# Two buffers for moments and normalised x, q and k split a step sooner, operands made one by one, and weight sums on VectorE in an attention and mixer kernel

## The chip, the cores and the metric

The kernel runs on one core of a Trainium2 chip. What is measured is the device time of one execution, in microseconds. The profile and the trace are of one further execution that the hardware profiler recorded.

## What is computed

Three parts follow each other, in fp32: attention with normalised q and k over 4 batches and 12 heads (448 rows, 64 columns a head), then a block of two matrices with a ReLU between them behind a layer norm, then the same kind of block behind a low-rank mixing along the rows.

```python
q_n, k_n = rmsnorm(q, g_q), rmsnorm(k, g_k)
attn = softmax(q_n @ k_n.T / sqrt(64))                 # 48 heads of 448 x 448
x = (attn @ v)                                         # as 4 x 448 x 768
xn = (x - mean) / sqrt(var + 1e-06) * g_ln
x = x + relu(xn @ w_ch1) @ w_ch2                       # 768 -> 3072 -> 768
u = x + (x.transpose(0, 2, 1) @ U @ V).transpose(0, 2, 1)   # rank 32
out = u + relu(u @ w_ch1b) @ w_ch2b
```

## The kernel before, in words

**Attention.** Two heads are a pair; there are 24 pairs, six for a batch, and each pair is worked in four steps n = 4t + i of 112 rows, so there are 96 steps and 6 that drain. TensorE's order in a step is fixed: the scores of step n (L643), for both heads the product with v of step n - 2 (L663) and the transposes of the exponentials of step n - 1 (L651); after them, where i = 2, the transposes of the next pair's normalised K (L631, `turn_k`), and in some steps those of a finished x or of a normalised x (L674, `turn_x`). All transposes go to two scratch banks in PSUM, sc_ps, taken in turn; the engine that reads a bank frees it. ScalarE copies the first head's transposes, makes the exponentials, and splits q and k (`q_high`, `k_high`: the part that fits the faster matmul format; the rest is q_lo and k_lo, and a product takes three matmuls, hi x hi, hi x lo, lo x hi). VectorE takes the maximum (L951), multiplies it into a bias (L957), makes k_lo (L943) where i = 3, copies the second head's transposes (L962), and does the sums for the norms. GpSimd squares q and k (L517, `squares`, where i = 3), takes the power -1/2 (L523, `root`, i = 0), scales K and makes q_lo (`norm_k` and `q_low`, i = 2). x of a pair stays in one of seven buffers until the statistics of its batch's six pairs are combined (`aggregate`, L990, on VectorE, where i = 3 of the pair after the batch's last), a root is taken (`root_var`) and GpSimd or, at the end, VectorE has normalised it (`normalise`). `XN_AT` says in which step a normalised x is transposed; ScalarE scales it into st_n (`keep_norm`) and SyncE stores it in HBM as xnrm.

**The four stages.** Stages 0 and 1 are the first block for two batches each, stages 2 and 3 the second. A stage has 156 products in a list `prods` (the steps end as the list begins): six times two groups of seven (kind "G", L696) and twelve of kind "M" (L706). The seven products P1 to P7 multiply sums of quarters of the weights by sums of quarters of the input (the scheme of Strassen and Winograd), and VectorE combines them. A product's weights are split by ScalarE (`weight_high`, four products ahead) and VectorE (`weight_low`, three ahead). Four of a group's seven need a sum of weights, made by GpSimd at places given by `sums_at`, five, five, four and zero products before, from the group's first: L579. For the first group of all, these places fall between the attention's last steps: the list `seq` has ("pre", -5) after step 58 and ("pre", -4) after step 59.

**Making operands.** Before a stage its input is loaded as three sets of four quarter tiles (c = 0 to 2: into `make0` in stage 0, into make_a, make_b and ht after), and from each set GpSimd makes four differences in place, ScalarE seven high parts (in_hi) and VectorE seven low parts (in_lo, L1012). `make_at` lays these out: ten consecutive places a set, of which the first is the load of all four tiles, which share one semaphore. For stage 0 the places begin at steps 66, 77 and 88 less the two of the load; for the others at the last M's first product, and 3 and 5 after it. In stages 1 and 2 the low-rank mixing runs beside the products, in twelve items, six for each pair of batches, 22 products apart from the tenth product on (`MIX_FROM`): load, transposes, products, and a store that the loads of stage 2 and 3 wait for.

What sets the order is each engine's own queue: every engine walks the list `seq` and issues what its own block puts at a place, and semaphores do the rest. The waits that the change touches are these:

```python
def aggregate(b):                                  # VectorE
    wait(dve, norm_done, PB * b)                   # moments has one buffer
def keep_norm(t):                                  # ScalarE
    wait(act, xn_out, 16 * t)                      # st_n has one buffer
def load_made(s, c):                               # SyncE, stages 2 and 3
    sp.wait_ge(mx_out, 32 * ITEMS * (s - 1))       # all of the mixing
```

## Time and profile before

| | us |
|---|---|
| median of 3 runs | 1830.38 (1827.22 to 1836.04) |
| the profiled execution, time | 1818.59 |
| its span in the trace | 1816.8 |
| PE busy in the span | 1772.3 (98%) |
| DVE busy | 1121.1 (62%) |
| ACT busy | 683.0 (38%) |
| POOL busy | 495.3 (27%) |

PE is TensorE, DVE VectorE, ACT ScalarE, POOL GpSimd and SP SyncE, whose queue issues the DMAs. Times in the trace count from the span's start. A busy TensorE need not be one at its peak: it runs at 2.4 or at 1.2 GHz, and the granted clock, 1.00 or 0.50 or between them in a stretch that has both, stands beside the windows. "[3.35 <-DVE e_t L962]" behind an instruction means that its engine sat idle so long before it and what ended that. L with a number is a line of the kernel.

### The profile page before, as it was taken

Reading aid. Unit: us, or ns where it says so; the run is one execution under the profiler, and the core shown is the slowest. Engines: PE = TensorE matmul, PEld = TensorE weight load, DVE = VectorE, ACT = ScalarE, POOL = GpSimd, SP = SyncE. Lnnn points to the kernel's source line nnn. Section 1 sums busy time; section 2 is a strip of 40 time slices with the busy share of each in tenths; the row PEclk is TensorE's granted clock in tenths of the full one; section 3 lists DMA queues with packets and bytes.
Section 4 is the critical chain, followed back from the end, with each engine's and each line's share of the span. In section 5 each row is a group of like instructions: output and inputs, shape, how many; then the busy total and the mean of one; then the engine's idle time right before and its main releaser. Section 6 shows DMA issues by size and latency. Waiting matters only on the chain.

```text
span 1816.8 us, 27033 instructions
## 1 busy us (share of the span) xinstructions
PE 1772.3 (98%) x9972; PEld 1598.1 (88%) x9972; DVE 1121.1 (62%) x2088; ACT 683.0 (38%) x1588; POOL 495.3 (27%) x419
## 2 busy tenths in 40 slices
PE   9999999999999999999999998999999989999999
PEld 8888777878999999899998897998888979999998
DVE  5787655586555565865655568566545694555554
ACT  4666544465233322433222334333223242333221
POOL 5556664364111111411110115111111151011110
PEclk9999965588999999999999999999999999999999
DMA  3222221221221211432222214322222252212112
GB/s 110 65 79 78 72 87 57 72 77 66 66 88 63 70 53 53 164 135 89 73 73 73 73 62 160 138 73 74 71 73 73 78 182 91 70 53 70 46 59 79
DMA packets 54738, 149.28 MB, mean 82 GB/s; under 512 B 5984, under 2 KB 36832, under 8 KB 54608
## 3 DMA queue, kind: packets, MB, share of 16 engines
q1 hardware_dynamic: 54608, 147.55, 24.7%
q8 instruction: 81, 1.33, 0.3%
q14 instruction: 49, 0.40, 0.1%
HBM read 122.75 MB, written 24.77 MB: 81 GB/s over the span
## 4 chain that ended last, share of the span: by engine, by line
PE 87%; DVE 8%; POOL 2%; DMA 1%; issue 1%; ACT 1%; SPq 0%; DVEq 0%; ACTq 0%; POOLq 0%
PE mm_ps L706 35%; PE mm_ps L696 31%; PE mm_ps L663 9%; PE mm_ps L643 4%; PE sc_ps L651 4%; DVE in_lo L1012 3%; PE sc_ps L674 1%; POOL x_nat L586 1%; DVE acc L1052 1%; DVE w_lo L1003 1%; PE sc_ps L718 1%; POOL qk_sq L517 1%; PE mm_ps L743 1%; DMA xres<-xa 1%; DVE h_lo L1019 1%
## 5 line engine op out<-in xcount | busy, mean ns | idle before, releaser
L706 PE MATMUL mm_ps<-h_hi,w_hi 128*128 128x448 f32 x1152 | 424.0, 368 | 10.3 <-DVE w_lo L1003 9.7
L706 PE MATMUL mm_ps<-h_hi,w_lo 128*128 128x448 f32 x1152 | 421.6, 366 | 0.0
L706 PE MATMUL mm_ps<-h_lo,w_hi 128*128 128x448 f32 x1152 | 421.6, 366 | 0.0
L1052 DVE TENSOR_TENSOR acc<-mm_ps,acc 128x448 f32<-128x448 f32 x288 | 166.3, 619 | 364.1 <-PE mm_ps L706 364.1
L696 PE MATMUL mm_ps<-in_hi,w_hi 128*128 128x448 f32 x1008 | 372.1, 369 | 2.3 <-DVE w_lo L1003 1.2
L696 PE MATMUL mm_ps<-in_hi,w_lo 128*128 128x448 f32 x1008 | 368.5, 366 | 0.0
L696 PE MATMUL mm_ps<-in_lo,w_hi 128*128 128x448 f32 x1008 | 368.4, 365 | 0.0
L825 ACT ACTIVATE w_hi<-w_raw 128x256 fp32r<-128x256 f32 (+1 forms) x480 | 205.7, 452 | 212.8 <-PE mm_ps L706 187.7
L706 PEld LDWEIGHTS mm_ps<-h_hi,w_hi 128*128 128x128 f32 x1152 | 216.5, 188 | 29.8 <-DVE w_lo L1003 11.6
L706 PEld LDWEIGHTS mm_ps<-h_hi,w_lo 128*128 128x128 f32 x1152 | 216.7, 188 | 17.8
L706 PEld LDWEIGHTS mm_ps<-h_lo,w_hi 128*128 128x128 f32 x1152 | 216.8, 188 | 17.3
L1003 DVE TENSOR_TENSOR w_lo<-w_raw,w_hi 128x256 fp32r<-128x256 f32 (+1 forms) x480 | 231.0, 493 | 0.2
L663 PEld LDWEIGHTS mm_ps<-v,e_t 112*112 112x112 f32 x1536 | 192.3, 202 | 34.7 <-issue 27.1
L663 PE MATMUL mm_ps<-v,e_t 112*112 112x64 f32 x1536 | 209.4, 287 | 0.0
L696 PEld LDWEIGHTS mm_ps<-in_hi,w_hi 128*128 128x128 f32 x1008 | 189.6, 188 | 18.9 <-DVE w_lo L1003 3.7
L696 PEld LDWEIGHTS mm_ps<-in_hi,w_lo 128*128 128x128 f32 x1008 | 189.5, 188 | 15.4
L862 ACT ACTIVATE h_hi<-ht 128x448 fp32r<-128x448 f32 x144 | 83.4, 579 | 317.1 <-DVE ht L1037 175.2
L696 PEld LDWEIGHTS mm_ps<-in_lo,w_hi 128*128 128x128 f32 x1008 | 189.6, 188 | 14.4
L579 POOL TENSOR_TENSOR w_s<-w_raw 128x384 f32<-128x384 f32 x48 | 57.5, 1198 | 501.9 <-DMA w_raw<-in_w 431.9
L579 POOL TENSOR_TENSOR w_s<-w_raw,w_s 128x384 f32<-128x384 f32 x48 | 49.4, 1029 | 506.7 <-DVE w_lo L1003 506.7
L791 ACT ACTIVATE e_nat<-mm_ps,nbias,rs 112x448 f32<-112x448 f32 x192 | 136.9, 722 | 6.6 <-DVE nbias L957 6.6
L951 DVE TENSOR_REDUCE nmax<-mm_ps 112x2 f32<-112x896 f32 x96 | 104.7, 1091 | 52.2 <-PE mm_ps L643 51.4
(104 smaller groups left out, 2040.1 us busy)
## 6 DMA issues: line engine op xcount, KB each, us to landing
w_raw<-in_w SPq DMA_DIRECT2D x96, 768.0 KB, 4.4
qk<-in_qkv SPq DMA_DIRECT2D x24, 448.0 KB, 3.8
acc<-xres SPq DMA_DIRECT2D x6, 1344.0 KB, 9.7
qt_raw<-in_q_t SPq DMA_DIRECT2D x24, 224.0 KB, 2.5
v<-in_qkv SPq DMA_DIRECT2D x24, 224.0 KB, 2.6
xnrm<-st_n SPq DMA_DIRECT2D x24, 224.0 KB, 1.9
xres<-acc SPq DMA_DIRECT2D x24, 224.0 KB, 2.2
xa<-xres SPq DMA_DIRECT2D x24, 224.0 KB, 2.7
```

The lines of the kernel that those rows point to most:

```text
L579: nc.gpsimd.tensor_tensor(out, in0, in1, op).then_inc(sum_done, 1)
L643: last = nc.tensor.matmul(mm_ps[:TP, 2 * (n % 2) + h, :S], a[rows, t % 2, i * TP:(i + 1) * TP], b[rows, t % 2], start=a is q_hi and b is k ...
L651: last = nc.tensor.transpose(to[:TP, c * TP:(c + 1) * TP], e_nat[:, n % 3, h, c * TP:(c + 1) * TP], ident[:TP, :TP])
L663: last = nc.tensor.matmul(mm_ps[:TP, 4 + t % 2, cols], e_t[h][:, c * TP:(c + 1) * TP], v[:, t % 2, h, c], start=c == 0, stop=c == NI - 1)
L696: last = nc.tensor.matmul(bank(q), w[a][:, c * P:(c + 1) * P], x[:, k, c], start=k not in ONTO and c == 0 and p == 0, stop=c == HC - 1 and ...
L706: last = nc.tensor.matmul(bank(q, b), w[a][:, c * P:(c + 1) * P], x[:, half, 2 * c + b], start=half == 0 and c == 0 and p == 0, stop=half ...
L791: nc.scalar.activation(e_nat[:, n % 3, h], mm_ps[:TP, 2 * (n % 2) + h, :S], ACT.Exp, bias=nbias[:, n % 2, h:h + 1], scale=rs[:, t % 2, 0, ...
L825: nc.scalar.activation(w_hi[:, q % RING, :width(q)], weights(q), ACT.Copy).then_inc(whi_done, 1)
L862: nc.scalar.activation(h_hi[:, g % 2, h], src, ACT.Relu).then_inc(hhi_done, 1)
L951: nc.vector.reduce_max(nmax[:, n % 2], mm_ps[:TP, 2 * (n % 2):2 * (n % 2) + 2, :S], axis=AX, negate=True).then_inc(max_done, 1)
L1003: nc.vector.tensor_tensor(w_lo[:, q % RING, :w], weights(q), w_hi[:, q % RING, :w].bitcast(F32), ALU.subtract).then_inc(wlo_done, 1)
L1052: nc.vector.tensor_tensor(acc[:, b, d], bank(q, b), acc[:, b, d], ALU.add).then_inc(ev_done, 1)
```

## The change

Several things are changed together. moments, var4 and rstd4 have two buffers by the batch's parity, and the waits are for the batch before the last. st_n has two buffers with a semaphore each. `XN_AT` has the transposes of normalised x only in steps with i = 0 or 1. `q_high` is issued at i = 1 instead of 2, and `k_high` at the end of i = 2 instead of the start of i = 3; `root_var` and `normalise` follow the buffers. `make_at` is replaced by four lists, one each for loads, sums, highs and lows: each tile has its own load and semaphore, each sum its own place, and for stage 0 no high part is made at i = 3. For stages 1 to 3 the order in which operands are made is P1, P7, P5, P3, P2, P6, P4, and the places spread from 10 products before the last M to 11 after. The loads of stages 2 and 3 wait for the mixing item that wrote their tile alone. `MIX_FROM` is 4 instead of 10, and the wait for all low parts before a mixing item is gone. The sums of weights are issued by VectorE at the same places, `weight_sum` ahead of `weight_low`. The shortened diff:

```diff
-    make_at = {}
-    for c, first in enumerate((66, 77, 88)):
-        for off in range(-2, 8):
-            make_at.setdefault(("step", first + off + off // 3), []).append((0, c, off))
+    MADE = ((P1, P3, P2, P5, P7, P6, P4), (P1, P7, P5, P3, P2, P6, P4))
+    load_made_at, sum_made_at, high_made_at, low_made_at = {}, {}, {}, {}
+    slots = [n for n in range(65, N) if n % NI != NI - 1][:7 * HC]
+    for c in range(HC):
+        at = slots[7 * c:7 * c + 7]
+        for k, n in zip(MADE[0], at):
+            high_made_at.setdefault(("step", n), []).append((0, c, k))
+            low_made_at.setdefault(("step", n + (n % NI == 2)), []).append((0, c, k))
+        for k, n in ((P5, at[1]), (P7, at[1]), (P6, at[2]), (P4, at[3])):
+            sum_made_at.setdefault(("step", n), []).append((0, c, k))
+        for tile in range(4):
+            n = 63 if c == 0 else slots[7 * c - 7 + (3, 4, 6, 5)[tile]] + 1
+            load_made_at.setdefault(("step", n), []).append((0, c, tile))
     for s in range(1, STAGES):
         first = number["M", s - 1, NJ - 1, 0]
-        for c in range(HC):
-            for off in range(-2, 8):
-                make_at.setdefault(("prod", first + (0, 3, 5)[c] + off), []).append((s, c, off))
-    MIX_FROM, MIX_STEP, ITEMS = 10, 22, 2 * HC
+        for c, ats in enumerate(((-5, -3, -1, 1, 2, 4, 6), (-4, -2, 0, 2, 3, 6, 10), (5, 7, 8, 8, 9, 10, 11))):
+            for k, n in zip(MADE[1], ats):
+                high_made_at.setdefault(("prod", first + n - 1), []).append((s, c, k))
+                low_made_at.setdefault(("prod", first + n), []).append((s, c, k))
+            for k, n in ((P5, ats[0]), (P7, ats[0]), (P6, ats[3]), (P4, ats[4])):
+                sum_made_at.setdefault(("prod", first + n), []).append((s, c, k))
+            for tile in range(4):
+                load_made_at.setdefault(("prod", first + (-10, -8, 2)[c]), []).append((s, c, tile))
+    MIX_FROM, MIX_STEP, ITEMS = 4, 22, 2 * HC
...
-            XN_AT[4 * (PB * (b + 1) + 2) + ((0, 4, 8, 12, 16, 20), (0, 2, 4, 6, 8, 10), (0, 4, 8, 12, 14, 16))[b][c]] = t
+            XN_AT[4 * (PB * (b + 1) + 2) + ((0, 4, 8, 12, 16, 20), (0, 1, 4, 5, 8, 9), (0, 4, 8, 12, 13, 16))[b][c]] = t
...
-                def load_made(s, c):
+                def load_made(s, c, n):
+                    b, cc = 2 * (s % 2) + n % 2, c + n // 2 * HC
                     if s == 0:
-                        sp.wait_ge(xn_out, 16 * (PB + HC + c + 1))
+                        u = PB * b + cc
+                        sp.wait_ge(xn_out[u % 2], 16 * (u // 2 + 1))
                         if c:
-                            sp.wait_ge(inlo_done[c - 1], made(0, P4))
+                            sp.wait_ge(inlo_done[c - 1], made(0, (P5, P7, P4, P6)[n]))
+                            sp.wait_ge(tin_done[c - 1], 4)
                     else:
+                        sp.wait_ge(inlo_done[c], made(s - 1, P4))
...
-                            sp.wait_ge(mx_out, 32 * ITEMS * (s - 1))
-                            sp.wait_ge(inlo_done[c], made(s - 1, P4))
+                            sp.wait_ge(mx_out, 32 * (ITEMS * (s - 2) + HC * (n % 2) + cc // 2 + 1))
                         if c == 2:
                             sp.wait_ge(hlo_done, 4 * NG * s)
+                    sp.dma_start(make_tiles(s, c)[:, n], (xnrm if s < 2 else xres)[b, cc]).then_inc(make_in[c][n], 16)
...
-                                all_made(sp, prods[n][1] + 1)
...
                 def root_var(b):
                     pool.wait_ge(var_done, b + 1)
-                    nc.gpsimd.tensor_tensor(rstd4[:], var4[:], m_half[:TP, :NI], ALU.pow).then_inc(rstd_done, 1)
+                    wait(pool, norm_done, PB * (b - 1))
+                    nc.gpsimd.tensor_tensor(rstd4[:, b % 2], var4[:, b % 2], m_half[:TP, :NI], ALU.pow).then_inc(rstd_done, 1)
...
+                def make_sum(s, c, k):
                     b11, b12, b21, b22 = (make_tiles(s, c)[:, x] for x in range(4))
+                    for n in {P5: (0, 1), P7: (3,), P6: (), P4: (2,)}[k]:
+                        pool.wait_ge(make_in[c][n], 16 * (s + 1))
+                    wait(pool, tin_done[c], 4 * s + SUMS.index(k))
+                    if k in (P5, P6, P4):
+                        pool.wait_ge(inlo_done[c], made(s, {P5: P1, P6: P3, P4: P2}[k]))
+                    out, in0, in1 = {P5: (b11, b12, b11), P7: (b12, b22, b12), P6: (b22, b22, b11),
+                                     P4: (b21, b21, b22)}[k]
+                    nc.gpsimd.tensor_tensor(out, in0, in1, ALU.subtract).then_inc(tin_done[c], 1)
...
-                            for u in (xn_pair(n + 1), xn_pair(n + 3)):
+                            for u in (xn_pair(n + 1), xn_pair(n + 2)):
...
-                    wait(act, xn_out, 16 * t)
-                    nc.scalar.activation(st_n[:], scratch("n", t)[:, :S], ACT.Copy,
+                    wait(act, xn_out[t % 2], 16 * (t // 2))
+                    nc.scalar.activation(st_n[t % 2][:], scratch("n", t)[:, :S], ACT.Copy,
...
-                        if i == 3 and t + 1 < NP_:
-                            k_high(t + 1)
...
+                        if i == 1 and t + 1 < NP_:
+                            q_high(t + 1)
                         if i == 2 and t + 1 < NP_:
-                            q_high(t + 1)
+                            k_high(t + 1)
...
-                    wait(dve, norm_done, PB * b)
+                    wait(dve, norm_done, PB * (b - 1))
...
+                def weight_sum(r, k):
+                    weights_in(dve, r)
...
+                    nc.vector.tensor_tensor(out, in0, in1, op).then_inc(sum_done, 1)
...
+                    for r, k in sums_at.get(n, ()):
+                        weight_sum(r, k)
                     for q in low_at.get(n, ()):
                         weight_low(q)
```

## Rows read from the trace of the kernel before

**Rows 1.** The page's 40 slices of the span: granted TensorE clock in tenths.
```profile
PEclk9999965588999999999999999999999999999999
```

**Rows 2.** Windows of attention: from:to, length, busy (xinstructions) by engine, granted clock, DMA.
```profile
14.00:200.00 186.00, 184.05 (x1681) 155.62 (x1680) 142.35 (x283) 122.09 (x302) 109.70 (x77) 1.00 0.25 74
...
201.50:208.50 7.00, 5.32 (x28) 4.54 (x29) 4.70 (x12) 2.59 (x6) 2.85 (x1) 0.53 0.00 1
...
235.30:265.80 30.50, 30.05 (x151) 25.03 (x149) 13.47 (x26) 14.14 (x34) 20.76 (x21) 0.50 0.28 84
265.80:280.40 14.60, 12.21 (x112) 10.36 (x110) 10.78 (x22) 8.95 (x21) 6.95 (x4) 0.97 0.36 105
280.40:355.10 74.70, 74.62 (x377) 63.66 (x377) 39.59 (x76) 32.12 (x77) 25.32 (x17) 0.50 0.19 57
355.10:389.50 34.40, 30.88 (x286) 26.36 (x284) 31.59 (x53) 22.94 (x55) 27.17 (x22) 0.99 0.28 85
389.50:399.30 9.80, 9.75 (x48) 7.95 (x48) 3.81 (x6) 5.04 (x13) 6.21 (x6) 0.50 0.17 59
...
409.40:418.90 9.50, 9.45 (x48) 7.93 (x48) 3.40 (x5) 4.82 (x13) 9.42 (x12) 0.50 0.07 24
```

**Rows 3.** Timeline, full clock, steps 42 and 43: start, duration, engine, line, idle before.
```profile
164.41 0.55 PE L631 MATMUL sc_ps<-ident,qk_sq 112*128 112x112 f32 x4
...
164.92 0.60 DVE L962 COPY e_t<-sc_ps 112x448 f32<-112x448 f32 x1
...
165.79 1.09 DVE L951 TENSOR_REDUCE nmax<-mm_ps 112x2 f32<-112x896 f32 x1 [0.27 <-PE mm_ps L643]
...
166.92 0.21 DVE L957 TENSOR_TENSOR nbias<-nmax,rs 112x2 f32<-112x2 f32 x1
167.06 0.67 DVE L943 SCALAR_TENSOR_TENSOR k_lo<-sc_ps,g_qk,k_hi 128x448 fp32r<-128x448 f32 x1
167.08 1.89 POOL L517 TENSOR_TENSOR qk_sq<-qk 112x1024 f32<-112x1024 f32 x1
...
167.88 0.57 PE L651 MATMUL sc_ps<-ident,e_nat 112*112 112x112 f32 x4
```

**Rows 4.** Timeline of step 51, where VectorE aggregates the second batch's moments.
```profile
201.46 0.84 DVE L994 BATCH_NORM_AGGREGATE moments<-stats 112x2 f32<-112x36 f32 x4 [4.45 <-POOL x_nat L586]
...
203.18 0.97 PE L651 MATMUL sc_ps<-ident,e_nat 112*112 112x112 f32 x4 [3.35 <-DVE e_t L962]
```

**Rows 5.** Timeline of step 59, after the first two sums of weights.
```profile
232.31 0.99 POOL L579 TENSOR_TENSOR w_raw<-w_raw 128x384 f32<-128x384 f32 x1
232.32 1.00 DVE L957 TENSOR_TENSOR nbias<-nmax,rs 112x2 f32<-112x2 f32 x1
...
234.06 0.57 PE L651 MATMUL sc_ps<-ident,e_nat 112*112 112x112 f32 x4 [1.98 <-DVE k_lo L943]
```

**Rows 6.** Timeline of step 87, VectorE beside GpSimd.
```profile
386.90 1.88 POOL L517 TENSOR_TENSOR qk_sq<-qk 112x1024 f32<-112x1024 f32 x1
...
386.92 1.88 DVE L957 TENSOR_TENSOR nbias<-nmax,rs 112x2 f32<-112x2 f32 x1
```

**Rows 7.** Windows at the three changes of stage, columns as in rows 2.
```profile
735.00:790.00 55.00, 52.60 (x258) 47.78 (x257) 49.52 (x74) 25.13 (x55) 25.60 (x20) 1.00 0.57 199
1080.00:1150.00 70.00, 64.86 (x316) 58.53 (x315) 58.39 (x91) 28.62 (x65) 25.59 (x20) 1.00 0.55 188
1435.00:1484.00 49.00, 43.94 (x208) 39.39 (x207) 39.07 (x58) 21.19 (x47) 18.76 (x15) 0.97 0.44 141
```

**Rows 8.** Groups by form on VectorE: count, busy us and mean ns, idle before.
```profile
L1052 DVE TENSOR_TENSOR acc<-mm_ps,acc 128x448 f32<-128x448 f32 x288 | 166.3, 619 | 364.1 <-PE mm_ps L706 364.1
...
L1003 DVE TENSOR_TENSOR w_lo<-w_raw,w_hi 128x384 fp32r<-128x384 f32 x192 | 108.8, 567 | 0.0
...
L1012 DVE TENSOR_TENSOR in_lo<-make_a,in_hi 128x448 fp32r<-128x448 f32 x21 | 26.9, 1282 | 12.3 <-ACT in_hi L838 12.3
```

**Rows 9.** Groups by form, GpSimd, columns as in rows 8.
```profile
L579 POOL TENSOR_TENSOR w_s<-w_raw 128x384 f32<-128x384 f32 x48 | 57.5, 1198 | 501.9 <-DMA w_raw<-in_w 431.9 <-DVE w_lo L1003 70.0
```

More of the change, by code:

```diff
@@ L458, in _ @@
                             emptied(sp, "n", u)
-                            sp.dma_start(xnrm[u // PB, u % PB], st_n[:]).then_inc(xn_out, 16)
-                        for s, c, off in make_at.get((what, n), ()):
-                            if off == -2:
-                                load_made(s, c)
+                            sp.dma_start(xnrm[u // PB, u % PB], st_n[u % 2][:]).then_inc(xn_out[u % 2], 16)
+                        for s, c, tile in load_made_at.get((what, n), ()):
+                            load_made(s, c, tile)
                     if what != "step":
@@ L477, in _ @@
                             emptied(sp, "n", u)
-                            sp.dma_start(xnrm[u // PB, u % PB], st_n[:]).then_inc(xn_out, 16)
-                        for s, c, off in make_at.get((what, n), ()):
-                            if off == -2:
-                                load_made(s, c)
+                            sp.dma_start(xnrm[u // PB, u % PB], st_n[u % 2][:]).then_inc(xn_out[u % 2], 16)
+                        for s, c, tile in load_made_at.get((what, n), ()):
+                            load_made(s, c, tile)
                         if n in store_at:
@@ L888, in _ @@
                             keep_norm(xn_pair(n - 1))
-                        for s, c, off in make_at.get((what, n), ()):
-                            make_high(s, c, off)
+                        for s, c, k in high_made_at.get((what, n), ()):
+                            make_high(s, c, k)
                         if 0 <= n - 1 < N:
@@ L911, in _ @@
                             hidden_high(g, C21)
-                        for s, c, off in make_at.get((what, n), ()):
-                            make_high(s, c, off)
+                        for s, c, k in high_made_at.get((what, n), ()):
+                            make_high(s, c, k)
                         if (at := mix_of(n)):
@@ L1004, in weight_low, with make_low @@
                                             ALU.subtract).then_inc(wlo_done, 1)
-                def make_low(s, c, off):
-                    if not 1 <= off <= 7:
-                        return
-                    k = MADE[off - 1]
+                def make_low(s, c, k):
                     dve.wait_ge(inhi_done[c], made(s, k))
@@ L1091, in _ @@
                             aggregate(t // PB - 1)
-                        for s, c, off in make_at.get((what, n), ()):
-                            make_low(s, c, off)
+                        for s, c, k in low_made_at.get((what, n), ()):
+                            make_low(s, c, k)
                         if 0 <= n - 1 < N:
@@ L1110, in _ @@
                             hidden_low(g, C21)
-                        for s, c, off in make_at.get((what, n), ()):
-                            make_low(s, c, off)
+                        for s, c, k in low_made_at.get((what, n), ()):
+                            make_low(s, c, k)
                         if (at := mix_of(n)):
```

114 lines of the change are left out of this document (44 added, 70 removed).

## The prediction

> **What bounds the kernel now.** I read the page's slices first. TensorE has the full clock (2.4 GHz) in almost all of them and the half one (1.2 GHz) in a part of slices 5 to 8, which is the second half of attention [rows 1]. From about 435 us on TensorE is busy nearly everywhere: there the matmuls are the bound, and what the change moves between other engines there is off the path. So I then cut the attention and the stage changes into windows. Until 200 us TensorE is idle for 186 - 184.05 = 1.95 us and keeps the full clock. After that come five stretches at half clock, of 7.0, 30.5, 74.7, 9.8 and 9.5 us, 131.5 us together [rows 2]. In the longest TensorE starts 377 matmuls in 74.7 us, 5.05 per us, against 1681 in 186 us, 9.04 per us, before: the mix of work is much the same, so about 44% of such a stretch is lost, 57.9 us in all. The timeline tells what stood ahead of the falls. In step 51 VectorE sits 4.45 us until GpSimd has normalised the last x of the batch before, since moments has one buffer; TensorE idles 3.35 us [rows 4]. In step 59 VectorE's bias product takes 1.00 us instead of 0.2 because GpSimd is summing weights, k_lo comes late and TensorE idles 1.98 us [rows 3, 5]. In the full-clock windows while operands are made, TensorE is idle 14.6 - 12.21 = 2.4 and 34.4 - 30.88 = 3.5 us [rows 2]. The three changes of stage hold 2.4, 5.1 and 5.1 us of idle TensorE, and the last also a clock of 0.97 [rows 7]; VectorE is short there: in_lo from make_a means 1.28 us where w_lo of nearly the same size takes 0.57 [rows 8].
>
> **The change, part by part.** Times are against the profiled execution, 1818.6 us, which is 11.8 us below the median of the runs shown.
>
> **Two buffers for moments.** VectorE's aggregation in step 51 then waits for the batch before the last, long done. The idle 3.35 us goes, and the 7.0 us of half clock behind it (44%: 3.1 us). Gain 6.4 us. What is late next in that step is nothing: VectorE has its 0.84 us of aggregation as it has elsewhere.
>
> **Turns of normalised x, two stages for them, q_hi and k_hi sooner.** The transposes of normalised x leave the steps in which K is transposed. There they took a scratch bank, so that the first transposes of the next step, and not the second, needed K's bank emptied. That gives k_lo the time of one more product with v and one more group of transposes. q_hi one step sooner lets q_lo run before K's transposes; then the squares on GpSimd start when these end instead of 167.08 - 164.96 = 2.1 us later [rows 3]. The squares take 1.89 us, and the bias product began 1.96 us after the transposes, so they just miss it; in step 87 they ran together and the bias product took 1.88 us, to the end of the squares [rows 6]. The row says that VectorE gets no part of its work done until GpSimd's instruction is over. The Trainium skill ("SBUF — State Buffer", "Who interferes with whom") says that a VectorE instruction with two inputs in SBUF contends with a GpSimd instruction that reads SBUF, and that the second to issue fully blocks; by that rule the new sums on VectorE are blocked by squares as well, and the trace agrees, with 1.88 us.
>
> **Sums of weights on VectorE.** 192 sums leave GpSimd (1.0 to 1.2 us each [rows 5, 9]) and cost about 0.57 us each on VectorE, by w_lo of the same shape [rows 8], some 109 us. In the stages VectorE has 364 us of waiting for TensorE's products in the accumulation alone [rows 8], and each sum stands four to five products before its matmul, so I count nothing. If that cover went, it would show as TensorE waiting for w_lo. But the first two, P5 and P7 of the first group, stand between steps 58 and 59. VectorE's copy ends 165.52 - 164.96 = 0.56 us after K's transposes [rows 3]; the squares now started with the end of these and hold the first sum until 1.9 us after it; with 0.57 us for each sum VectorE reaches the maximum at 3.0 us or later, where it now starts at 0.83. k_lo then is 2.2 us late or more, TensorE has 0.15 us of slack [rows 3], and behind the waiting transposes the whole queue of TensorE stands. That is 2.0 us of idle. Bounds: 0.7 us if nothing blocks the sums (0.56 + 2 x 0.57 - 0.83 - 0.15), 3.9 us if the second sum and the bias product each wait behind another GpSimd instruction of about the 1 us of [rows 5]. I take 3.0, since GpSimd goes on to normalising at once and one such wait is what both [rows 5] and [rows 6] show. It stands where 1.98 us are idle now, and as now a half-clock stretch will follow; its length isn't tied to anything I can name, so I take the mean of the five, 26.3 us, loss 11.6. Before: 1.98 + 0.44 x 30.5 = 15.4 us; after: 14.6. Gain 0.8 us.
>
> **Operands for the first stage, made singly.** Highs and sums leave the crowded steps, loads go tile by tile; no low part is made any more in a step in which VectorE has the statistics. Before, the stretches behind step 67 (74.7 + 9.8 + 9.5 = 94 us) cost 41.4 us and the idle 5.9, 47.3 together. One crowded place is left: steps 66 and 67, where two sums stand before the squares while GpSimd has eight normalisations behind it. I keep one stretch of 10 us (4.4) and 3 us of idle. Gain 40 us. Bounds: nothing (the stretches come back as long), and 47.3.
>
> **Changes of stage.** Mixing starts six products sooner, so its last store, and behind it on SyncE the loads of the quarter tiles, come sooner: 8 and 9 products for make_a and make_b (10 and 8 before the last M's first product instead of 2 before and 1 after), one for ht, and the waits are per tile. The 21 in_lo spread over 17 products instead of 12. Eight sums of weights (4.6 us) come into VectorE there, and it loses about as many blocked waits. The queue behind SyncE's new wait for the last mixing store is the load of the next weights, five products later, covered. Idle and clock now: 12.6 us, and 0.03 x 49 x 2 = 2.9 us at half clock, 1.3: 13.9 together. I keep 3, gain 11. Bounds: a loss of 3, a gain of 13.9. The shift of the mixing against the products I count at zero, with 2 us either way.
>
> Sum: 6.4 + 0.8 + 40 + 11 = 58.2, so 1818.6 - 58.2 = 1760.4 for an execution like the profiled one. The unprofiled runs lie higher now, and if that is half clock, a third of it should stay: I add 4, **1764 us**.
>
> **Rivals.** (1) The clock never falls: the squares or the sums in step 59 are passed more cheaply. For it: 200 us with 1.95 us of idle and full clock [rows 2]. Against it: the blocked sum above. It gives 1818.6 - 6.4 - 15.4 - 47.3 - 13.9 = 1736, with some small idle 1740.
> (2) The falls are only rearranged: short idle keeps bringing them, and half clock lasts as long as now. For it: the longest stretch has 0.08 us of idle in 74.7, so being busy does not bring the clock back soon [rows 2]. The gain is 3.35, half of the 5.9 and 11 at the stages: 1801, and 1811 for a run as high as the others now. The Trainium skill ("TensorE: Matmul & The Clock Gate", "A second HAM failure mode: psum-queue depth-cycling") has a rule for this side: frequent short idle times between groups of matmuls make the clock go to and fro. Only in part does the trace agree, since 1.95 us of such idle in 186 us did no harm.
> (3) No change that counts: late loads or VectorE close the stage changes no better and half clock grows a little: 1815 to 1827.
> (4) Slower, by one mechanism: the blocked sum before step 59 takes the clock down and it stays down until the products begin. Of 235.3 to 418.9 us, 124.5 are at half clock now and 59.1 not; their 53.2 busy us would take 53.2 / 0.56 = 95, 36 more than the 59.1. That gives 1818.6 - 6.4 + 36 - 11 = 1837. It decides once the stretch behind step 59 is longer than about 150 us.
>
> **Chances.** Forecast 0.47, rival 1 0.18, rival 2 0.22, rival 3 0.09, rival 4 0.04. The range from 1740 to 1808 holds the forecast, nearly all of rival 1 and most of rival 2, with the bounds of the stage changes inside. About 0.5% (9 us) is what a measurement of this kernel can tell from no change: faster by more is forecast and rivals 1 and 2, 0.87; within it 0.09; slower 0.04.
>
> **What would show it.** Right: no wait of the aggregation for x_nat; the two sums between steps 58 and 59 stretched beside qk_sq, with 2 to 4 us of idle TensorE in step 59 and half clock behind; after that at most 40 us of half clock; w_s rows on VectorE near 570 ns and in_lo nearer 700 than 1282; under 2 us of idle at each change of stage; first products some 45 us sooner. Wrong: half clock of 100 us or more, a new wait of TensorE for w_lo in the stages, or TensorE waiting for in_lo.

## The result, and the profile after

The changed kernel takes 1766.17 us in the median of 4 runs (1761.03 to 1781.51), the kernel before on the same chip 1828.80 (1812.04 to 1836.04): ratio 0.968, 95% interval 0.9604 to 0.9757, 62.6 us less. The forecast was 1764. Here and below, medians and ranges are of all runs, while ratios and their intervals leave out the runs that took over 1.5% longer than the fastest of the same kernel. The profiled execution is the slowest of the four, 1781.5 us with a span of 1779.7; its mean granted clock is 0.971, that of the others 0.981 to 0.985. So the trace of after shows more half clock than its median has.

The page, engines and clock by slices (span 1779.7 us), to set against [rows 1]:

```profile
PE 1752.5 (98%) x9972; PEld 1586.9 (89%) x9972; DVE 1154.1 (65%) x2280; ACT 679.1 (38%) x1588; POOL 297.2 (17%) x227
...
PEclk9999979569999999999999999999999999999999
```

GpSimd lost 198 us of work, VectorE gained only 33 (it has the 107 us of sums and is blocked less). Cut where the clock changes, the attention of after reads as follows (columns as in [rows 2]):

```profile
14.00:200.00 186.00, 184.51 (x1697) 157.07 (x1696) 149.14 (x292) 123.19 (x304) 111.67 (x78) 1.00 0.25 74
...
226.50:250.30 23.80, 22.68 (x114) 19.57 (x116) 12.23 (x26) 11.65 (x28) 12.47 (x11) 0.50 0.33 104
250.30:311.80 61.50, 57.34 (x525) 48.18 (x522) 51.71 (x104) 44.15 (x106) 43.56 (x33) 1.00 0.29 90
311.80:390.30 78.50, 78.50 (x398) 67.43 (x399) 40.75 (x76) 34.48 (x81) 43.58 (x38) 0.50 0.18 55
```

There are two stretches at half clock (1.2 GHz), 102 us together, where [rows 2] had five and 131.5. The first one came out near its forecast, 23.8 us against 26.3. The second, 78.5 us, was not forecast: after it "at most 40 us" was to be left. With 102 us, this execution even meets one of the prediction's own signs of being wrong, "half clock of 100 us or more". In both stretches TensorE is busy for nearly all of the time, so being busy does not bring the full clock back soon.

**Step 51**, where [rows 4] had the wait: VectorE now aggregates without waiting.

```profile
195.95 0.83 DVE L976 BATCH_NORM_AGGREGATE moments<-stats 112x2 f32<-112x36 f32 x4
```

**Ahead of the first stretch**, step 59, the timeline (start, duration, engine, line, idle before); it answers [rows 5]:

```profile
222.64 2.62 POOL L532 TENSOR_TENSOR qk_sq<-qk 112x1024 f32<-112x1024 f32 x1 [1.64 <-PE sc_ps L616]
...
222.97 0.55 DVE L1002 TENSOR_TENSOR w_s<-w_raw 128x384 f32<-128x384 f32 x1
...
223.62 2.06 DVE L1002 TENSOR_TENSOR w_raw<-w_raw 128x384 f32<-128x384 f32 x1
...
225.60 1.08 DVE L933 TENSOR_REDUCE nmax<-mm_ps 112x2 f32<-112x896 f32 x1
...
227.62 0.97 PE L636 MATMUL sc_ps<-ident,e_nat 112*112 112x112 f32 x4 [2.29 <-DVE k_lo L925]
```

The first sum of weights gets through in 0.55 us and the squares take 2.62 instead of 1.89; the second sum then takes 2.06 us and ends at 225.68, 0.4 us after the squares (225.26). So the maximum starts at 225.60, and behind it the bias product and k_lo, and TensorE is idle 2.29 us.

**Ahead of the second stretch**, step 78, same columns:

```profile
301.50 3.21 POOL L538 TENSOR_TENSOR rs<-qk_ms,m_half 112x16 f32<-112x16 f32 x1 [5.34 <-DVE qk_ms L921]
...
304.67 1.00 POOL L555 TENSOR_TENSOR rstd<-var,m_half 112x4 f32<-112x4 f32 x1
...
305.65 3.62 POOL L566 TENSOR_TENSOR make<-make 128x448 f32<-128x448 f32 x3
...
309.23 1.05 POOL L543 TENSOR_TENSOR qk_sq<-qk,rs 112x512 f32<-112x512 f32 x1
...
310.33 0.60 PE L616 MATMUL sc_ps<-ident,qk_sq 112*128 112x112 f32 x4 [2.66 <-POOL qk_sq L543]
```

This is GpSimd's own queue. Behind the root of the pair stand the root of the batch's variances and three differences for the second set of operands (P5 and P7 placed at step 76, P6 at 77); only then comes the scaling of K that TensorE's transposes of step 78 need. The prediction looked at VectorE and at steps 66 and 67, where the idle is 0.69 us, and not at this queue.

**Changes of stage**, to set against [rows 7]:

```profile
712.00:767.00 55.00, 54.56 (x272) 50.23 (x271) 46.76 (x86) 24.99 (x58) 12.15 (x8) 1.00 0.53 183
1058.00:1128.00 70.00, 69.17 (x345) 63.47 (x344) 57.39 (x104) 30.44 (x70) 16.01 (x12) 1.00 0.48 167
1410.00:1459.00 49.00, 49.00 (x244) 45.42 (x242) 44.29 (x77) 21.78 (x50) 16.06 (x12) 1.00 0.45 146
```

Idle is 0.4, 0.8 and 0.0 us, 1.3 together, where it was 12.6. Some of it moved: the summary of TensorE's waits has for before, and then for after (engine, line, releaser: us in total, times, longest):

```profile
PE sc_ps L718 <- DVE xs_lo L1058: 10.2, 16, 1.3
PE mm_ps L706 <- DVE w_lo L1003: 9.7, 5, 3.2
...
PE mm_ps L696 <- DVE w_lo L1003: 1.2, 2, 0.6
```

```profile
PE sc_ps L703 <- DVE xs_lo L1059: 9.8, 16, 0.9
...
PE sc_ps L721 <- DVE mix L1063: 2.3, 5, 0.6
```

The waits for w_lo are gone, a small one in the mixing is new. VectorE's groups by form answer [rows 8] and [rows 9]:

```profile
L1053 DVE TENSOR_TENSOR acc<-mm_ps,acc 128x448 f32<-128x448 f32 x288 | 166.2, 618 | 331.7 <-PE mm_ps L691 331.7
...
L1007 DVE TENSOR_TENSOR w_lo<-w_raw,w_hi 128x384 fp32r<-128x384 f32 x192 | 105.4, 549 | 0.1
...
L1002 DVE TENSOR_TENSOR w_raw<-w_raw 128x384 f32<-128x384 f32 x48 | 28.3, 590 | 5.0
L1002 DVE TENSOR_TENSOR w_s<-w_raw 128x384 f32<-128x384 f32 x48 | 26.4, 549 | 0.0
...
L1013 DVE TENSOR_TENSOR in_lo<-make_a,in_hi 128x448 fp32r<-128x448 f32 x21 | 17.7, 844 | 0.0
```

**A cut that the clock blurs little.** The products begin after all half clock of attention. Their first row splits a span into two parts:

| profiled execution | first product at | from there to the end | half clock ahead of it | half clock behind it |
|---|---|---|---|---|
| before | 431.6 | 1385.2 | 133 | 3 |
| after | 409.6 | 1370.1 | 102 | 0 |
| before, idle filled (b_fill) | 382.8 | 1384.1 | 0 | 10 |
| after, idle filled (z_fill) | 369.4 | 1370.8 | 0 | 0 |

The last two columns are sums over windows of 1 us each, without the last 2 us of a span; what stands behind the first product lies at changes of stage. The first products, of before, after, b_fill and z_fill:

```profile
431.61 0.45 PE L696 MATMUL mm_ps<-in_hi,w_hi 128*128 128x448 f32 x1
```

```profile
409.58 0.45 PE L681 MATMUL mm_ps<-in_hi,w_hi 128*128 128x448 f32 x1
```

```profile
382.84 0.45 PE L696 MATMUL mm_ps<-in_hi,w_hi 128*128 128x448 f32 x1
```

```profile
369.41 0.45 PE L681 MATMUL mm_ps<-in_hi,w_hi 128*128 128x448 f32 x1
```

So the products are 15.1 us shorter. The first product comes 22.0 us sooner, where the prediction had some 45. How much shorter attention is at full clock is known only roughly. The two filled kernels differ by 13.4 us, but b_fill has more dummies, and they take longer than the idle they stand in for (an estimate from 0.12 us a record: 21 us of them for some 12 us of idle, in z_fill 7 for 5). The two unfilled ones give 22.0 - 0.44 x 31 = 8 us. The rest of the 62.6, some 34 to 39 us, is half clock that no longer comes, or comes for less long.

### The profile page after: what moved, and what is told of

The parts are those of the page before. It is cut to its first block, busy times and chain, and to the rows that moved or that the text cites. A ratio compares the mean times of both kernels' runs of the same rounds, so it can differ in the third digit from the quotient of the medians.

```text
span 1779.7 us, 27087 instructions
## 1 busy us (share of the span) xinstructions
PE 1752.5 (98%) x9972; PEld 1586.9 (89%) x9972; DVE 1154.1 (65%) x2280; ACT 679.1 (38%) x1588; POOL 297.2 (17%) x227
## 4 chain that ended last, share of the span: by engine, by line
PE 79%; DVE 2%; issue 1%; ACT 0%; POOL 0%; DVEq 0%; ACTq 0%
PE mm_ps L691 39%; PE mm_ps L681 32%; PE mm_ps L648 3%; PE sc_ps L636 1%; PE mm_ps L628 1%; PE sc_ps L703 1%; PE sc_ps L713 1%; PE sc_ps L659 1%; DVE h_lo L1020 0%; ACT h_hi L844 0%; PE sc_ps L721 0%; DVE xs_lo L1059 0%; DVE ht L1030 0%; DVE ht L1040 0%; DVE w_lo L1007 0%
## 5 line engine op out<-in xcount | busy, mean ns | idle before, releaser
L648 PEld LDWEIGHTS mm_ps<-v,e_t 112*112 112x112 f32 x1536 | 187.6, 197 | 33.4 <-issue 28.0
L648 PE MATMUL mm_ps<-v,e_t 112*112 112x64 f32 x1536 | 204.8, 283 | 0.0
L681 PEld LDWEIGHTS mm_ps<-in_hi,w_hi 128*128 128x128 f32 x1008 | 189.3, 188 | 14.8 <-issue 0.2
L566 POOL TENSOR_TENSOR make_a<-make_a 128x448 f32<-128x448 f32 x12 | 14.7, 1226 | 940.8 <-DVE in_lo L1013 940.4
L810 ACT ACTIVATE w_hi<-w_s 128x384 fp32r<-128x384 f32 x144 | 72.6, 516 | 210.3 <-DVE w_s L1002 210.2
```

Of the source, the lines that this page charges most:

```text
L648: last = nc.tensor.matmul(mm_ps[:TP, 4 + t % 2, cols], e_t[h][:, c * TP:(c + 1) * TP], v[:, t % 2, h, c], start=c == 0, stop=c == NI - 1)
L681: last = nc.tensor.matmul(bank(q), w[a][:, c * P:(c + 1) * P], x[:, k, c], start=k not in ONTO and c == 0 and p == 0, stop=c == HC - 1 and ...
L810: nc.scalar.activation(w_hi[:, q % RING, :width(q)], weights(q), ACT.Copy).then_inc(whi_done, 1)
```

## The experiments

The theory: idle of TensorE brings the half clock, through two queues, VectorE's in step 59 and GpSimd's in step 78. The rivals were that the half clock comes by itself or from the load, that the sums of weights matter in the stages, and that one part of the change does it all. Ratios are to the kernel before, run on the same chip: its medians were 1840.65 (u_wait to u_wsum), 1828.71 (x_sums to x_both_wait), 1835.02 (z_fill, y_pre, y_wsum) and 1831.04 us (b_fill). Where no other kernel is named, an edit is made to the changed one. The groups ran on different chips, so a difference of medians between groups is rough, and the ratios are the fairer comparison; the changed kernel's is 0.968 (0.9604 to 0.9757).

### One part of the change undone

**u_wait**: the aggregation waits for the batch just before again.

```diff
-                    wait(dve, norm_done, PB * (b - 1))
+                    wait(dve, norm_done, PB * b)
```

> The changed kernel with one edit undone: VectorE's aggregation waits for all of the batch before again. Theory (idle TensorE brings half clock): idle of 3 to 3.5 us in step 51 is back, and a half-clock stretch right behind it, so some 6 us or more over the changed kernel: 1770 to 1785. Rival (half clock comes by itself, whatever the idle): the idle comes back alone, the clock near 200 us stays full, and the time is within 4 us of the changed kernel's 1766.

Measured: 1792.03 us (1767.98 to 1814.49), ratio 0.9681 (0.9546 to 0.9816). The wait is back, 2.5 us of VectorE, but TensorE idles only 1.42 us for it and in the profiled run the clock did not fall there. It fell in step 59, behind 2.31 us, and stayed down (the third of the long stretches below). So the expectation, a stretch right behind step 51, was missed, and the ratio, which leaves out two of the four executions, is that of the changed kernel: this run alone does not settle what the wait costs.

**u_turns**: the steps of the transposes of normalised x, and the places of `q_high`, `k_high` and `normalise`, as before.

```diff
-            ... (0, 1, 4, 5, 8, 9), (0, 4, 8, 12, 13, 16))[b][c]] = t
+            ... (0, 2, 4, 6, 8, 10), (0, 4, 8, 12, 14, 16))[b][c]] = t
+                        if i == 3 and t + 1 < NP_:
+                            k_high(t + 1)
...
-                        if i == 1 and t + 1 < NP_:
+                        if i == 2 and t + 1 < NP_:
                             q_high(t + 1)
-                        if i == 2 and t + 1 < NP_:
-                            k_high(t + 1)
```

> The changed kernel with the turns of normalised x at i = 2 again and q and k split a step later, as before. Theory: k_lo is late by 1 to 2 us wherever K and normalised x are transposed in one step (steps 58, 62, 66, 94), more idle TensorE from step 59 on and more half clock: 1775 to 1800. Rival (the turns are hidden, sums and operands did it all): 1762 to 1770.

Measured: 1810.05 us (1790.67 to 1847.89), ratio 0.9773 (0.9667 to 0.9879). TensorE idles 2.07 us in step 59 and 1.61 in a later step, and the clock is down in between and long after. The ratio's interval overlaps that of the changed kernel, so what this part is worth is not settled.

**u_stage**: the changes of stage laid out as before (`MIX_FROM` 10, operands in their old order, loads and places late), but each tile by itself.

```diff
-    MADE = ((P1, P3, P2, P5, P7, P6, P4), (P1, P7, P5, P3, P2, P6, P4))
+    MADE = ((P1, P3, P2, P5, P7, P6, P4),) * 2
...
-    MIX_FROM, MIX_STEP, ITEMS = 4, 22, 2 * HC
+    MIX_FROM, MIX_STEP, ITEMS = 10, 22, 2 * HC
-        for c, ats in enumerate(((-5, -3, -1, 1, 2, 4, 6), ...)):
+        for c, ats in enumerate((range(1, 8), range(4, 11), range(6, 13))):
...
-                load_made_at.setdefault(("prod", first + (-10, -8, 2)[c]), [])...
+                load_made_at.setdefault(("prod", first + (-2, 1, 3)[c]), [])...
```

> The changed kernel with the operands of stages 1 to 3 and the start of the mixing at their old places (per-tile loads and waits kept). Theory: VectorE is short again at the changes of stage, though less, since sums of weights no longer stretch in_lo from GpSimd's side: 5 to 12 us of idle TensorE there in place of 1.3, time 1771 to 1779. Rival (weight sums leaving GpSimd closed the gaps, not the places): under 3 us of idle, 1764 to 1769.

Measured: 1770.20 us (1762.97 to 1787.96), ratio 0.966 (0.9548 to 0.9771). The median says nothing, since these runs happened to have less half clock (0.976 to 0.990 granted). The cut does: first product at 382.4, from there to the end 1384.9 us, 14.8 more than after and as much as before. The waits for w_lo are back, 6.4 us in 8 places.

**u_wsum**: all sums of weights on GpSimd again.

```diff
                 def weight_sum(r, k):
-                    weights_in(dve, r)
+                    weights_in(pool, r)
...
-                    nc.vector.tensor_tensor(out, in0, in1, op).then_inc(sum_done, 1)
+                    nc.gpsimd.tensor_tensor(out, in0, in1, op).then_inc(sum_done, 1)
```

> The changed kernel with all sums of weights on GpSimd again. Theory: nothing in the stages (TensorE's products bound them), and in step 59 idle TensorE falls from 2.3 us to about 1 since VectorE reaches its maximum in time and only the bias product meets GpSimd; 1755 to 1768. Rival (the move to VectorE is what pays, by ending contention in the stages): w_lo and in_lo stretched, over 5 us of idle in the changes of stage, 1772 or more.

Measured: 1755.95 us (1742.15 to 1761.89), ratio 0.955 (0.9467 to 0.9634), some 10 us *below* the changed kernel by the medians, 24 by the ratios. In the profiled run no idle over 0.61 us and no half clock stand between the first steps and step 78; what is left is step 78, 2.65 us and 10 us of half clock. The products take 1371.7 us, 1.6 more. So in the stages it hardly matters who sums the weights, and in step 59 VectorE is the wrong place.

The long stretches, windows of the three profiled runs of u_turns, x_sums (below) and u_wait:

```profile
228.70:413.00 184.30, 182.18 (x915) 155.37 (x916) 93.50 (x177) 79.60 (x188) 81.07 (x62) 0.50 0.21 63
```

```profile
227.60:406.00 178.40, 178.39 (x903) 152.57 (x903) 91.52 (x177) 78.61 (x187) 81.64 (x62) 0.50 0.21 65
```

```profile
229.60:408.00 178.40, 178.36 (x902) 152.55 (x903) 92.38 (x177) 78.47 (x187) 81.53 (x62) 0.50 0.22 65
```

The last two have 0.01 and 0.04 us of idle TensorE in 178 us and stay at half clock.

### The two queues mended

**x_sums**: the differences for the first stage's operands go to other steps, so that none stands ahead of the scaling of K.

```diff
-        for k, n in ((P5, at[1]), (P7, at[1]), (P6, at[2]), (P4, at[3])):
+        for k, n in zip((P5, P7, P6, P4), ((67, 67, 70, 71), (75, 75, 78, 79), (85, 85, 86, 88))[c]):
```

> The changed kernel with the first stage's differences moved: P5 and P7 of sets 0 and 1 behind the squares (steps 67 and 75), P6 and P4 behind K's transposes. Theory: norm_k in step 78 is no longer behind three differences and a root, the 2.66 us of idle there and 0.5 us in step 74 go, and with them the stretch of half clock behind them; the stretch behind step 59 stays. Profile with under 50 us of half clock, time 1740 to 1755. Rival (half clock comes by itself): same half clock as the changed kernel, 1760 to 1768.

Measured: 1757.36 us (1751.73 to 1812.31), ratio 0.9622 (0.9558 to 0.9686). The profiled run is the slowest: the 2.30 us of step 59 were followed by the 178 us above, so the expectation, under 50 us of half clock, was missed. No idle of step 78 is left in it, but at half clock there is none in u_wait either, where the queue is as it was. That the edit removes it is shown by x_both and y_pre, where TensorE reaches step 78's transposes at full clock and does not wait.

**x_pre**: the sums of weights of the very first group move out of the squares' way.

```diff
-            for k, at in ((P5, -5), (P7, -5), (P6, -4), (P3, 0)):
+            for k, at in ((P5, -4), (P7, -3), (P6, -2), (P3, 0)) if r == 0 else (...as before...):
```

> The changed kernel with the first group's sums spread over the places behind steps 59, 60 and 61 instead of two behind 58 and one behind 59. Theory: VectorE reaches the maximum of step 59 in time, idle TensorE there falls from 2.3 us to under 0.8, and the half-clock stretch at 227 to 250 us goes, about 10 us; the later one stays: 1750 to 1760. Rival: the stretch is there all the same, within 4 us of 1766.

Measured: 1744.72 us (1741.70 to 1747.20), ratio 0.9568 (0.9509 to 0.9627), 21 below the changed kernel, and below the 1750 to 1760 expected. The 2.3 us of step 59 are gone, two of 0.90 and 0.94 us are there instead at 240 and 242, without a fall. Step 78 still idles 2.66 us, with 10 us of half clock behind it.

**x_both**: both edits.

> Both edits. Theory: no idle time of TensorE over 1 us from step 42 to the products, full clock through attention but for a few us at the start, 1730 to 1742. Rival: half clock of 60 us or more all the same, 1755 or more.

Measured: 1758.36 us (1740.96 to 1779.68), ratio 0.9603 (0.9543 to 0.9663). The expectation missed. The same pair of 0.9 us idles, which had full clock behind it in x_pre, now had 24 us of half clock, and GpSimd's queue struck in another way. The second idle of the pair and the window behind it, first of x_pre, then of x_both:

```profile
242.22 0.57 PE L636 MATMUL sc_ps<-ident,e_nat 112*112 112x112 f32 x4 [0.94 <-DVE k_lo L925]
```

```profile
242.30:260.00 17.70, 17.02 (x158) 14.45 (x158) 13.96 (x26) 13.21 (x32) 13.32 (x12) 1.00 0.34 111
```

```profile
242.49 0.97 PE L636 MATMUL sc_ps<-ident,e_nat 112*112 112x112 f32 x4 [0.94 <-DVE k_lo L925]
```

```profile
242.30:260.00 17.70, 17.51 (x88) 14.78 (x88) 7.42 (x14) 8.14 (x20) 9.48 (x9) 0.50 0.25 81
```

The timeline of x_both at step 78:

```profile
305.73 1.04 POOL L543 TENSOR_TENSOR qk_sq<-qk,rs 112x512 f32<-112x512 f32 x1
...
306.14 2.85 DVE L939 TENSOR_TENSOR nbias<-nmax,rs 112x2 f32<-112x2 f32 x1
...
306.74 1.14 POOL L549 TENSOR_TENSOR q_lo<-qt_raw,q_hi 128x448 fp32r<-128x448 f32 x1
...
307.83 1.15 POOL L566 TENSOR_TENSOR make<-make 128x448 f32<-128x448 f32 x1
...
311.17 0.57 PE L636 MATMUL sc_ps<-ident,e_nat 112*112 112x112 f32 x4 [1.82 <-DVE e_t L944]
```

The bias product (0.16 us when alone) takes 2.85 us: it begins under the scaling of K and ends at 308.99, with the third GpSimd instruction in a row (307.83 + 1.15 = 308.98). TensorE idles 1.82 us for it, and 55 us of half clock follow.

**x_both_wait**: x_both with u_wait's wait as well.

> Both edits, and the aggregation waiting for all of the batch before again, which puts one idle time of about 3.3 us into an attention part that has no other. Theory: exactly one half-clock stretch, from about 201 us, of 5 to 80 us; time 5 to 38 us over the kernel with both edits, and differing from run to run. Rival (a single idle time does nothing): 3 to 4 us over it and full clock.

Measured: 1780.18 us (1776.58 to 1813.66), ratio 0.9751 (0.969 to 0.9812), 22 us above x_both, 24 without the runs that the ratios leave out; the two intervals do not meet. Here the idle of step 51, 1.43 us, did have half clock behind it, 202 to 244. It was not the only stretch: behind 1.82 us of idle, as in x_both, stands another, 321 to 370.

### Idle taken away without taking the waits away

**z_fill**: the changed kernel, and dummy matmuls of the identity into unused columns, 14 in step 59 ahead of the second head's transposes and 16 in step 78 ahead of K's.

```diff
+                def fill(t, times):
+                    pe.wait_ge(xnat_done, t)
+                    for _ in range(times):
+                        nc.tensor.matmul(mm_ps[:, 4 + (t - 1) % 2, :P], ident[:], ident[:], start=True, stop=True)
...
+                            if n == 59 and h == 1:
+                                fill(14, 14)
                             if 0 <= n - 1 < N:
                                 turn_e(n - 1, h)
+                        if n == 78:
+                            fill(19, 16)
                         if n % NI == 2 and n // NI + 1 < NP_:
```

> The changed kernel, with every engine's work and waits as they are, but TensorE computes 14 products of the identity with itself while it waits in step 59 and 16 while it waits in step 78 (results unused, in a bank that is free). VectorE and GpSimd are as late as before. Theory (idle TensorE is what brings half clock): no stretch behind 228 us nor behind 310 us, full clock nearly throughout, 1735 to 1748, though the waits themselves stay. Rival (half clock comes by itself or from the other engines' load): stretches as in the changed kernel, 1760 to 1785.

Measured: 1742.40 us (1742.00 to 1790.04, 6 runs), ratio 0.9515 (0.9473 to 0.9556). Step 59 in the profiled run, timeline and window:

```profile
223.56 2.06 DVE L1011 TENSOR_TENSOR w_raw<-w_raw 128x384 f32<-128x384 f32 x1
...
225.10 3.34 PE L733 MATMUL mm_ps<-ident 128*128 128x128 f32 x28
...
228.28 0.55 PE L636 MATMUL sc_ps<-ident,e_nat 112*112 112x112 f32 x4
```

```profile
222.00:232.00 10.00, 10.00 (x95) 9.01 (x92) 8.28 (x14) 5.08 (x14) 9.43 (x9) 1.00 0.30 88
```

Each dummy shows as two records, so 14 as x28. The blocked sum takes 2.06 us as ever and the transposes start no sooner (228.28 against 227.62), but TensorE is not idle there and the clock does not fall in this execution: 24 us gained by matmuls whose results nobody reads. One run of six took 1790.04 at a clock of 0.969. No trace of it exists, so what brought its half clock is not known; in the profiled one the longest idle left is 1.56 us.

**b_fill**: the same on the kernel *before*, at ten places.

```diff
+                FILL = {(51, 0): 20, (59, 0): 12, (63, 0): 6, (67, 0): 8, (71, 1): 6, (75, 1): 6,
+                        (79, 1): 6, (83, 1): 7, (87, 1): 11, (91, 1): 6}
...
+                            if (n, h) in FILL:
+                                fill(n // NI, FILL[n, h])
```

> The kernel before with nothing moved: dummy identity matmuls into unused columns are put on TensorE ahead of the turn of e in steps 51, 59, 63, 67, 71, 75, 79, 83, 87 and 91, where it stood idle. All waits of the other engines stay. Theory (idle TensorE brings the half clock, whatever made it idle): the half clock shrinks from 134 us to under 60, and the time is 1770 to 1800 us with every wait of moments, of sums and of operands still there. Rival (the half clock comes by itself or from the load of the other engines, and the waits only stand beside it): half clock as before, 1820 to 1840 us.

Measured: 1768.67 us (1766.66 to 1783.86, 6 runs), ratio 0.9686 (0.9645 to 0.9726): as fast as the changed kernel, with nothing moved. The aggregation's wait for GpSimd is still there, as in [rows 4], beside the last of the dummies of step 51:

```profile
198.75 1.84 PE L751 MATMUL mm_ps<-ident 128*128 128x128 f32 x15
...
201.58 0.84 DVE L1004 BATCH_NORM_AGGREGATE moments<-stats 112x2 f32<-112x36 f32 x4 [4.46 <-POOL x_nat L586]
```

And three of the windows that were at 0.53, 0.50 and 0.50 in [rows 2]:

```profile
201.50:208.50 7.00, 7.00 (x68) 6.02 (x67) 6.11 (x15) 4.64 (x13) 2.46 (x1) 1.00 0.08 30
235.30:265.80 30.50, 28.48 (x259) 23.94 (x259) 22.79 (x45) 21.80 (x53) 25.26 (x24) 1.00 0.40 122
280.40:355.10 74.70, 73.66 (x675) 63.65 (x676) 67.06 (x119) 50.87 (x122) 50.43 (x38) 1.00 0.32 97
```

The engines beside TensorE work harder than before in the same windows (GpSimd 50.4 us against 25.3), and the clock stays full. That rules out, for these stretches, that load brings the half clock and that it comes by itself: all six runs have a clock of 0.992 or more, the eleven beside them of the kernel before 0.942 to 0.962. In the profiled run 10 us of half clock are left, all at changes of stage, behind two waits for w_lo of 3.17 us each.

### Versions meant to be faster

**y_pre**: x_pre, and the differences at steps (66, 66, 68, 69), (75, 75, 79, 79), (85, 85, 86, 88).

> First group's sums spread behind steps 59 to 61, and the second set's differences at steps 75 and 79 (behind the squares), none between root and K's transposes. Theory: idle in step 78 gone without a new long block of the bias product (that of step 78 waits at most for norm_k and q_low, 2 us, and idle TensorE under 1 us), so at most the pair of 0.9 us waits at 240 us is left: 1734 to 1745, under x_pre's 1744.7. Rival (what matters is chance, not place): 1745 to 1765 with falls at places without idle time over 1 us.

Measured: 1751.25 us (1738.20 to 1764.22), ratio 0.9553 (0.9498 to 0.9609). No better than x_pre, and above the 1734 to 1745 expected. In the profiled run half clock stands behind the pair of 0.90 and 0.94 us (10 us) and behind 0.71 and 0.47 us at 304 and 306 (48 us).

**y_wsum**: u_wsum with those same steps.

> All sums of weights on GpSimd, and the second set's differences at steps 75 and 79. Theory: the fall behind step 78's 2.65 us goes as well and none is left but by small idle times: 1734 to 1750, under u_wsum's 1756. Rival: the same time as u_wsum, 1751 to 1762.

Measured: 1742.15 us (1737.05 to 1742.65, 5 runs), ratio 0.9495 (0.946 to 0.9529): faster than both kernels, and with x_pre the steadiest version without dummies. Windows of its profiled run:

```profile
14.00:299.00 285.00, 280.40 (x2573) 238.23 (x2572) 234.99 (x457) 196.37 (x479) 192.12 (x141) 1.00 0.29 87
...
301.00:312.00 11.00, 10.73 (x56) 8.93 (x57) 5.85 (x10) 5.15 (x13) 7.83 (x6) 0.53 0.23 67
```

TensorE is idle 4.6 us in 285 and the clock is full; then 0.71 and 0.48 us close together bring 10 us of half clock.

## Why the prediction was right, and where it was not

**The direction, for the reason given.** It said that waits on TensorE's path are small in themselves and cost through the clock. b_fill and z_fill show this: at nearly full clock the two kernels differ by 1768.67 - 1742.40 = 26.3 us (31 by the ratios), where the measured difference is 62.6. So about half of the gain or more is half clock.

**That the median came out 2 us from the forecast is luck.** The largest term of the sum was far off (below). What made up for it was shorter half clock in the other runs than in the profiled one, 4 us more at the changes of stage, and the 4 us added.

**Moments, 6.4 us: the mechanism right, the size not fixed.** The wait is gone, and its idle and stretch with it. But with everything else of the change in place, what the single buffer costs differs: 22 us by x_both_wait against x_both, nothing certain by u_wait, whose ratio, 0.9681, is that of the changed kernel. Its own idle is then 1.4 us instead of 3.35; the rest is the stretch that may follow.

**Step 59, gain 0.8: right, by a chain that differed in one link.** Idle 2.29 against 3.0 taken, half clock 24 us against 26.3. The text had the squares hold the first sum; the row shows the first sum passing in 0.55 us, the squares lengthened by 0.7, and the second sum held. So "VectorE gets no part of its work done until GpSimd's instruction is over" holds for [rows 6] and not here. In the stages the sums cost nothing, as forecast: no wait for w_lo, 549 to 590 ns each against 570. That the length came out is luck: nearly the same idle in the same step was followed by 7 us in u_stage and 178 in u_wait and x_sums. "Its length isn't tied to anything I can name, so I take the mean" was the weak step. The mean of five stretches of one execution is no forecast of one; medians of several runs are needed, and the clock of each run is what to read.

**First-stage operands, 40 us: the step that failed.** "One crowded place is left: steps 66 and 67" was wrong. That place has 0.69 us of idle; the crowded one is step 78, where `root_var` and three differences stand ahead of `norm_k` in GpSimd's queue, 4.6 us of work. I had priced each moved instruction and not read the queue that it moved into. In the profiled executions half clock behind step 66 went from 94 to 78.5 us, a gain of some 7 us at 0.44, and idle went from 5.9 us to 4.2: 8.5 us together where 40 were counted. So the profiled execution lies 21 above the 1760.4 forecast for it. The other runs had a clock of 0.981 to 0.985, by 2 x (1 - 0.982) x 1765 some 64 us of half clock, and the median comes out at 1766.

**Changes of stage, gain 11: right, 15.1 measured** from the first product to the end, 14.8 by u_stage. Idle accounts for 12.6 - 1.3 = 11.3 and the clock's 0.97 for another 1.3; the last 2 to 3 us I did not find. in_lo from make_a came down from 1282 to 844 ns, less than the "nearer 700".

**The +4 for the median** had the wrong sign for this pair of executions: the profiled one before was 10 below its median and the profiled one after 15 above.

**The rivals.** (1), the clock never falls, 1736 to 1740: that was reached by no run of the changed kernel, but z_fill's 1742.0 and y_wsum's 1737.05 show that the price was right. (2), half clock as long as now, 1801 to 1811: u_turns comes nearest, with a median of 1810.05, and 184 us of half clock in its profiled run of 1821.0. The Trainium skill ("TensorE: Matmul & The Clock Gate", "A second HAM failure mode: psum-queue depth-cycling") has frequent short idle between groups of matmuls make the clock go to and fro. The runs agree in part: 0.71 and 0.48 us brought half clock in y_wsum, but the clock does not go to and fro, since one fall in attention lasts 7 to 184 us. (3), no change that counts, 1815 to 1827: the median is 49 us under it. (4), the stretch behind step 59 lasts to the products, 1837: stretches over the named 150 us did come in variants (178 us in u_wait and x_sums, 184 in u_turns) and gave 1814, 1812 and 1821, not 1837. The rival put the extra half clock at 59 us; it was 178 - 133 = 45, and the 8 to 13 us that attention gained at full clock and the 15.1 of the products stood against it. (Its 53.2 busy us left out 1.1 us of idle at 399.3 to 409.4 us; that moves it by 2 us.) The mechanism was real and did not decide the sign.

**What stays open.** Which idle has a fall behind it. In attention all of 1.8 us and more at full clock did, in every profiled run (1.82 to 3.35 us), and none of 0.6 us and less did by itself. At the changes of stage even the long ones differ: of before's two longest waits for w_lo, the 3.18 us at 1480 had 3 us of half clock behind it and the 3.19 us at 1121 none (timeline and window of before):

```profile
1121.25 0.47 PE L706 MATMUL mm_ps<-h_hi,w_hi 128*128 128x448 f32 x1 [3.19 <-DVE w_lo L1003]
```

```profile
1121.00:1129.00 8.00, 7.17 (x34) 6.34 (x35) 8.00 (x15) 1.93 (x4) 2.33 (x2) 1.00 0.67 213
```

Between 0.6 and 1.8 us both happened, for the same instructions: a pair of 0.9 us had no fall in x_pre and one in x_both and y_pre; 1.42 had none in u_wait and 1.43 had one in x_both_wait. Nor is it known what ends a stretch: within the long ones TensorE was as busy as it can be. Both make the time of one execution a draw, and none of my edits could steer that, only take occasions away.

## What to carry to other kernels

Where TensorE is nearly always busy and the granted clock falls, look for the idle of one to three microseconds just ahead of each fall, and price it by the half clock behind it, not by itself; a few dummy matmuls at that place tell whether the idle is the cause, and may be a cure as good as the rearrangement. Before work is moved off a busy engine, write down the queue of the engine that it moves to, step by step, around the one instruction that TensorE waits for. Take several runs of each kernel, since one may have 7 us of half clock and the next 178. And compare parts of the trace that the clock hardly blurs (here first product to end) before trusting medians that differ by less than their spread.

## What I had not expected of the hardware

- Being fully busy does not restore the clock: 78.5 us with no idle at all, and 178.4 us with 0.01, at 1.2 GHz throughout.
- Keeping TensorE fed with work that has no use is worth 62 us (1831.04 to 1768.67) on the kernel before.
- A blocked two-input VectorE instruction does not get in between two GpSimd instructions that follow each other closely: 2.85 us through three of them in x_both. The Trainium skill ("SBUF — State Buffer", "Who interferes with whom") has an exclusive lock on a shared port pair, and the second to issue blocked. The traces agree in part: the second sum took 2.06 us beside the squares and the bias product in x_both waited for more than one instruction, but the first sum, issued 0.33 us after the squares, got through in 0.55.
- The blocking goes both ways: the squares took 2.62 us instead of 1.89 when a sum on VectorE ran beside their start.
